# Block attention, experts and FFN on one core: host-made windows of keys and values, block means by VectorE and GpSimd

## What is computed

```python
B, H, S, D = q.shape
block, window = (32, 16)
nb = S // block                                   # 24
k_sum = k.reshape(B, H, nb, block, D).max(axis=3)
v_sum = v.reshape(B, H, nb, block, D).mean(axis=3)
scores_l = scale * np.matmul(q, k.transpose(0, 1, 3, 2))
mask_l = np.abs(pos[:, None] - pos[None, :]) < window
scores_s = scale * np.einsum('bhsd,bhnd->bhsn', q, k_sum) + np.log(block)
scores_all = np.concatenate([np.where(mask_l, scores_l, -1e9), scores_s], axis=-1)
a = softmax(scores_all)                           # denominator + 1e-9
out = np.matmul(a, np.concatenate([v, v_sum], axis=2))
```

## Time and profile before

| what | value |
|---|---|
| runs | 876.49, 880.53, 880.81 us (median 880.53) |
| profiled execution | span 878.4 us; its own time is not listed apart from the three runs |
| PE busy | 855.3 us, 97% of the span |
| DVE, ACT, POOL busy | 248.8, 222.3, 226.6 us |
| the chain that ended last | PE 94%, DMA 4%, ACT 1% |
| DMA | 47.34 MB, mean 54 GB/s, nearly all of the first 70 us at full load |

### The profile page before, as it was taken

One profiled execution on the slowest core, in us unless ns is written; L12 is line 12 of the kernel. 1 busy time (PEld: TensorE's weight loads), 2 busy tenths in 40 slices (PEclk: granted clock), 3 DMA queues, 4 the chain that ended last, 5 costly groups with the idle time before them and its releaser, 6 DMA issues.

```text
span 878.4 us, 11397 instructions
## 1 busy us (share of the span) xinstructions
PE 855.3 (97%) x4224; PEld 709.1 (81%) x4224; DVE 248.8 (28%) x582; ACT 222.3 (25%) x494; POOL 226.6 (26%) x155
## 2 busy tenths in 40 slices
PE   5779999999999999999999999999999999999998
PEld 4668888888888888888888888888888888888886
DVE  4875412121212121212121211112333333333333
ACT  3665611112201012201022202032512133312121
POOL 2345712034502034502034502227510023300000
PEclk9999999999999999999999999999999999999999
DMA  9996350002200002200002200003200002010101
GB/s 213 234 227 150 110 213 0 1 5 97 90 1 0 0 24 96 72 0 0 0 24 96 72 0 0 0 0 119 73 0 0 0 24 72 1 48 0 48 0 48
DMA packets 41400, 47.34 MB, mean 54 GB/s; under 512 B 14944, under 2 KB 32416, under 8 KB 41248
## 3 DMA queue, kind: packets, MB, share of 16 engines
q1 hardware_dynamic: 39168, 45.94, 18.4%
q10 hardware_dynamic: 2208, 1.08, 0.6%
HBM read 42.76 MB, written 3.17 MB: 52 GB/s over the span
## 4 chain that ended last, share of the span: by engine, by line
PE 94%; DMA 4%; ACT 1%; DVE 0%; SPq 0%; issue 0%; ACTq 0%; POOL 0%; DVEq 0%; POOLq 0%
PE bank L761 30%; PE bank L762 30%; PE bank L763 30%; DMA v_win<-v_win 3%; PE bank L738 2%; PE bank L753 1%; PE bank L719 1%; DMA v_raw<-v_rows 1%; PE bank L729 1%; ACT prob L442 1%; SPq L269 0%; ACTq L456 0%; POOL q_bd L344 0%; ACT v_win L452 0%; DVE k_max L563 0%
## 5 line engine op out<-in xcount | busy, mean ns | idle before, releaser
L761 PE MATMUL bank<-x_hi,w_hi 128*128 (+1 forms) x576 | 225.7, 392 | 0.0
L762 PE MATMUL bank<-x_hi,w_lo 128*128 (+1 forms) x576 | 224.4, 390 | 0.0
L763 PE MATMUL bank<-x_lo,w_hi 128*128 (+1 forms) x576 | 224.2, 389 | 0.0
L626 DVE SCALAR_TENSOR_TENSOR h_lo<-bank,h_hi 128x512 fp32r<-128x512 f32 x96 | 66.4, 691 | 356.4 <-ACT h_hi L489 356.4
L761 PE MATMUL bank<-h_hi,w_hi 128*128 128x512 f32 x384 | 149.4, 389 | 0.0
L763 PE MATMUL bank<-h_lo,w_hi 128*128 128x512 f32 x384 | 149.4, 389 | 0.0
L762 PE MATMUL bank<-h_hi,w_lo 128*128 128x512 f32 x384 | 149.4, 389 | 0.0
L365 POOL TENSOR_TENSOR w_lo<-stage,w_hi 128x1024 fp32r<-128x1024 f32 x40 | 96.8, 2437 | 162.2 <-ACT w_hi L473 162.2
L489 ACT ACTIVATE h_hi<-bank 128x512 fp32r<-128x512 f32 x96 | 56.9, 592 | 313.9 <-PE bank L763 313.9
L391 POOL TENSOR_TENSOR x_acc<-x_acc,y_tmp 128x512 f32 (+1 forms) x48 | 60.5, 1297 | 262.1 <-DVE y_tmp L646 262.1
L761 PEld LDWEIGHTS bank<-x_hi,w_hi 128*128 128x128 f32 x576 | 108.1, 188 | 23.5 <-issue 0.8
(11 more groups left out here) (48 smaller groups left out, 601.7 us busy)
## 6 DMA issues: line engine op xcount, KB each, us to landing
stage<-weights SPq DMA_DIRECT2D x48, 512.0 KB, 3.3
v_win<-v_rows SPq DMA_DIRECT2D x8, 480.0 KB, 4.8
k_raw<-k_t SPq DMA_DIRECT2D x8, 384.0 KB, 6.4
q_bd<-q_t SPq DMA_DIRECT2D x16, 192.0 KB, 6.0
v_raw<-v_rows SPq DMA_DIRECT2D x8, 384.0 KB, 7.9
p_bc<-p_rows SPq DMA_DIRECT2D x1, 3072.0 KB, 9.9
out<-p_bc SPq DMA_DIRECT2D x12, 256.0 KB, 2.0
v_win<-v_win ACTq DMA_DIRECT2D x8, 132.0 KB
```

What stands on the lines that cost most here:

```text
L626: nc.vector.scalar_tensor_tensor(h_lo[:, f % NH, :], h_bank(cc, f)[:], 0.0, h_hi[:, f % NH, :].bitcast(F32), ALU.max, ALU.subtract).then_i ...
L761: nc.tensor.matmul(dst, w_h, a_h, start=first, stop=False)
L762: nc.tensor.matmul(dst, w_l, a_h, start=False, stop=False)
L763: return nc.tensor.matmul(dst, w_h, a_l, start=False, stop=last)
```

## The change

The host lays out windows of keys (with 24 zero columns behind each) and of values, and values with features in partitions. Cut to its core:

```diff
 # host
-        "k_t": features_first(k),
-        "v_rows": v_rows,
+        "k_w": np.pad(windows(k_rows), ((0, 0), (0, 0), (0, 0), (0, NBLK))),
+        "v_t": v_rows,                      # now features_first(v)
+        "v_w": np.ascontiguousarray(windows(v_rows).transpose(0, 3, 2, 1)),
 # SBUF
-            k_win = sb(att, "k_win", [P, 2, TILES, KEYS])
-            k_raw = sb(att, "k_raw", [P, 2, SEQ])
-            v_raw = sb(att, "v_raw", [P, 2, SEQ // P, P])
+            k_win = sb(att, "k_win", [P, NK, TILES, KEYS])      # NK = 3
+            v_cols = sb(att, "v_cols", [P, 2, SEQ])
+            v_sum = sb(att, "v_sum", [P, 2, NBLK])
 # SP: load_keys, load_value_columns, load_value_windows
-                wait_count(sp, kcopy_done, len(RUNS) * (u - 1))
-                sp.dma_start(k_raw[:, u % 2, :], k_t[u, :, :]).then_inc(k_in[u % 2], 16)
+                wait_count(sp, scores_done, GROUPS * (u - NK + 1))
+                sp.dma_start(k_win[:, u % NK, :, :], k_w[u, :, :, :]).then_inc(k_in[u % NK], 16)
...
                 wait_count(sp, vsum_done, u - 1)
-                sp.dma_start(v_raw[:, u % 2, :, :], v[u, :, :].rearrange("(t p) n -> p t n", p=P)
-                             ).then_inc(vraw_in[u % 2], 16)
+                sp.dma_start(v_cols[:, u % 2, :], v_t[u, :, :]).then_inc(vcols_in[u % 2], 16)
...
                 wait_count(sp, pv_done, GROUPS * (u - 1))
-                for t0, nt in RUNS:
...
-                    sp.dma_start(v_win[u % 2][0:KW, t0:t0 + nt, :], src).then_inc(v_in[u % 2], 16)
+                sp.dma_start(v_win[u % 2][0:KW, :, :], v_w[u, :, :, :]).then_inc(v_in[u % 2], 16)
...
             load_keys(0)
             load_queries(0)
             sp.dma_start(cst[:], consts).then_inc(const_in, 16)
+            load_value_columns(0)
+            load_value_windows(0)
             load_keys(1)
             load_queries(1)
-            load_values(0)
-            load_value_windows(0)
+            load_value_columns(1)
+            load_value_windows(1)
+            load_keys(2)
             sp.dma_start(dp[:], probs.rearrange("(p t) e -> p t e", p=P)).then_inc(dp_in, 16)
-            load_keys(2)
-            load_values(1)
             for u in range(2, UNITS):
+                load_queries(u)
+                load_value_columns(u)
                 if u + 1 < UNITS:
                     load_keys(u + 1)
-                load_queries(u)
-                load_values(u)
-                load_value_windows(u - 1)
+                load_value_windows(u)
                 load_weights(0, u - 2)
-            load_value_windows(UNITS - 1)
 # POOL, slot 3u+2, behind normalize and spread_key_maxima
+            def spread_value_means(u, slot):
+                pool.wait_ge(vmean_done, u + 1)
...
+                nc.gpsimd.tensor_copy(means[:, 1:TILES, :], means[:, 0:1, :].broadcast_to([NBLK, TILES - 1, P])
+                                      ).then_inc(vrep_done, 1)
+                pool.wait_ge(vrep_done, u + 1)
 # ACT, slot 3u+2
                 nc.scalar.activation(v_win[u % 2][KW:KEYS, 0, :], ps_v[KW:KEYS, 0:P], ACT.Copy
                                      ).then_inc(vmean_done, 1)
-                act.wait_ge(vmean_done, u + 1)
-                act.dma_start(means[:, 1:TILES, :], means[:, 0:1, :].broadcast_to([NBLK, TILES - 1, P])
-                              ).then_inc(vrep_done, 16)
 # DVE: maxima now from k_win; key_windows (slot 3u-1) gone; value_sums new in slot 3u+1
-            def key_windows(u):
...
+            def value_sums(u):
+                dve.wait_ge(vcols_in[u % 2], 16 * (u // 2 + 1))
+                wait_count(dve, vturn_done, u - 1)
+                nc.vector.tensor_reduce(v_sum[:, u % 2, :], v_cols[:, u % 2, :].rearrange("p (n j) -> p n j", j=BLOCK),
+                                        AXIS.X, ALU.add).then_inc(vsum_done, 1)
 # PE, slot 3u+2 (C_MEAN: identity / 32)
-                for t in range(SEQ // P):
...
-                    last = nc.tensor.matmul(ps_v[KW:KEYS, 0:P], cst[:, at:at + NBLK], v_raw[:, u % 2, t, :],
-                                            start=(t == 0), stop=(t == SEQ // P - 1))
+                nc.tensor.matmul(ps_v[KW:KEYS, 0:P], v_sum[:, u % 2, :], cst[:, C_MEAN:C_MEAN + P],
+                                 start=True, stop=True).then_inc(vturn_done, 1)
```

More of the change, by code:

```diff
@@ L60 @@
 SLOTS = ALL_GROUPS + L_X
[L63 to L73, removed]
+NK = 3
+C_ID, C_MEAN, C_MASK = 0, P, 2 * P
+C_ALL = C_MASK + 3 * KEYS
 def constants():
@@ L83, in constants, with attention_moe_ffn @@
         at = C_MASK + kind * KEYS
-        key = np.arange(KW)[None, :] + window_start(t) - QT * t
-        c[:, at:at + KW] = np.where(np.abs(query - key) < WINDOW, 0.0, MASKED / SCALE)
+        key = np.arange(KW)[None, :] - WINDOW
+        seen = (np.abs(query - key) < WINDOW) & (key + QT * t >= 0) & (key + QT * t < SEQ)
+        c[:, at:at + KW] = np.where(seen, 0.0, MASKED / SCALE)
         c[:, at + KW:at + KEYS] = np.log(BLOCK) / SCALE
-    for blk in range(P // BLOCK):
-        c[BLOCK * blk:BLOCK * (blk + 1), C_AVG + NBLK - P // BLOCK + blk] = 1.0 / BLOCK
+    c[:, C_MEAN:C_MEAN + P] = np.eye(P, dtype=np.float32) / BLOCK
     return c
-def attention_moe_ffn(nc, consts, q_t, k_t, v, probs, weights, p_rows, out):
+def attention_moe_ffn(nc, consts, q_t, k_w, v_t, v_w, probs, weights, p_rows, out):
     ctx = ExitStack()
@@ L149, in attention_moe_ffn @@
         q_zeroed_low = sem("q_zeroed_low")
-        k_in = [sem(f"k_in{s}") for s in range(2)]
+        k_in = [sem(f"k_in{s}") for s in range(NK)]
         q_in = [sem(f"q_in{s}") for s in range(2)]
-        vraw_in = [sem(f"vraw_in{s}") for s in range(2)]
+        vcols_in = [sem(f"vcols_in{s}") for s in range(2)]
         v_in = [sem(f"v_in{s}") for s in range(2)]
         kmax_done = sem("kmax_done")
-        kcopy_done = sem("kcopy_done")
         kwin_done = sem("kwin_done")
@@ L348, in spread_key_maxima @@
                 pool.wait_ge(kmax_done, u + 1)
-                wait_count(pool, scores_done, GROUPS * (u - 1))
-                nc.gpsimd.tensor_copy(k_win[:, u % 2, :, KW:KEYS],
+                nc.gpsimd.tensor_copy(k_win[:, u % NK, :, KW:KEYS],
                                       k_max[:, u % 2, :].unsqueeze(1).broadcast_to([P, TILES, NBLK])
                                       ).then_inc(kwin_done, 1)
+            def spread_value_means(u, slot):
+                pool.wait_ge(vmean_done, u + 1)
+                pool.wait_ge(norm_done, slot - L_NORM + 1)
+                pool.wait_ge(kwin_done, min(u + 1, UNITS - 1) + 1)
+                for f, half in split_half(slot - 1, 1):
+                    pool.wait_ge(wlo_done if half else wlo_half, f + 1)
+                means = v_win[u % 2][KW:KEYS, :, :]
+                nc.gpsimd.tensor_copy(means[:, 1:TILES, :], means[:, 0:1, :].broadcast_to([NBLK, TILES - 1, P])
+                                      ).then_inc(vrep_done, 1)
+                pool.wait_ge(vrep_done, u + 1)
             def normalize(k):
@@ L373, in split_half_lo @@
                                                w_hi[:, f, cols].bitcast(F32), ALU.subtract)
-                if half == 1:
-                    last.then_inc(wlo_done, 1)
+                last.then_inc(wlo_done if half else wlo_half, 1)
             for slot in range(SLOTS + 1):
@@ L383, in _ @@
                     spread_key_maxima(u)
+                for u in unit_starting(slot, L_MEAN):
+                    spread_value_means(u, slot)
                 for f, half in split_half(slot, 1):
@@ L672, in _ @@
                     key_maxima(u)
-                for u in unit_starting(slot, -1):
-                    key_windows(u)
+                for u in unit_starting(slot, 1):
+                    value_sums(u)
                 if slot == L_TRANS:
@@ L845, in features_first, with windows @@
                                     ).reshape(UNITS, P, SEQ)
-    v_rows = np.ascontiguousarray(v.reshape(BATCH, KT, 2, SEQ, DH).transpose(0, 1, 3, 2, 4)
-                                  ).reshape(UNITS, SEQ, P)
+    def windows(a):
+        padded = np.pad(a, ((0, 0), (0, 0), (WINDOW, WINDOW)))
+        return np.stack([padded[:, :, QT * t:QT * t + KW] for t in range(TILES)], axis=2)
+    k_rows, v_rows = features_first(k), features_first(v)
     halves = F2 // FE
@@ L868 @@
     out = nc.dram_tensor("out", (TOK, DM), F32, kind="ExternalOutput").ap()
-    attention_moe_ffn(nc, ap["consts"], ap["q_t"], ap["k_t"], ap["v_rows"], ap["probs"], ap["weights"],
+    attention_moe_ffn(nc, ap["consts"], ap["q_t"], ap["k_w"], ap["v_t"], ap["v_w"], ap["probs"], ap["weights"],
                       p_rows, out)
```

41 lines of the change are left out of this document (17 added, 24 removed).

## The result

| | runs, us | median | ratio to the kernel before, 95% interval |
|---|---|---|---|
| before | 876.49, 878.12, 880.53, 880.81 | 879.33 | |
| changed | 883.80, 884.33, 884.84, 885.33 | 884.59 | 1.0058 (1.0034 to 1.0081) |

The changed kernel is slower by 5.3 us. Its profiled execution has a span of 882.0 us and took 883.80, so 1.8 us lie outside the span; the spans differ by 3.6 us.

What follows compares the result with a forecast made beforehand. PE was taken as the bound, so only the first 105 us could move: -7.2 us by slot 19, -2.4 from units 6 and 7, +0.5 for half clock, rounded to -9: 880.5 - 9.0 = 871.5 us; range 866.5 to 880.

Steps and rivals of the forecast that it cites:

- the steps of the start: Start, unit 0: second keys' maxima at 14.3 instead of 9.57 us, ACT's copy done at 22.7 instead of 20.1, +2.6 us.
- the end of the wait for the spread: Values' wait for the DMA spreading means over v_win, 7.57 to 9.05 us of transfer, goes altogether.
- PE's means: Two matmul records replace twelve, 0.24 us instead of 1.42 a unit; sure for units 6 and 7, -2.4 us.
- the first landmark: End of unit 0's last values group: 30.8 us, against 28.2 before; 29.7 with a quicker spread and faster rows.
- GpSimd's copy: POOL's spread of means, 24 partitions by 1408 columns: 2.05 us, between 1.3 and 4.4.
- SP now blocks on values: SP's wait in load_value_windows(u) makes a loop through units 1 to 3: period 9.5 us, bounds 9.0 to 10.4.
- The queries' landing: In SP's loop, issue, windows, weights and queries: landed 6.8 us after values end, 8.2 if all at 230 GB/s.
- PE's three steps: Scores, transposing and values after the queries land, ending the unit: 2.2 us at full clock.
- The engines' own period: Time of a unit without a DMA wait, 9.0 us from the old kernel's last; lower bound of the loop.
- Queries come late: Rival, chance 0.07: landing takes 9.3 us, PE's next steps run at half clock, period 14.9; 890.6 us, slower.
- Only bytes count: Rival, chance 0.13: all DMA rows move at 233 GB/s, a unit takes 11.3 us; 879.6 us, no change.
- The spread is the wait: Rival, chance 0.10: POOL's copy needs 4.4 us, disturbed by DVE's reductions, period 10.5; 876.3 us.

Runs made afterwards that it cites:

- the fastest version: Changed kernel, second keys loaded ahead of first value columns and windows; SP's loop asks for windows(u-1) right after queries(u), ahead of keys: 866.79 us, ratio 0.9864.

## Why the prediction was wrong

**Right:** where the time is decided (before slot 19; PE without a gap from there but for 0.97 us), the steps of the start (maxima of unit 1 at 14.31 against 14.3, sums, first mask, spread, and ACT's copy done at 22.7 as added up), VectorE's prices, and the end of the wait for the spread. PE's means take 0.33 us a unit on the chain, not 0.24, so they save 1.1 and not 1.2.

That the first landmark came out at 30.77 against 30.8 is luck in part. Three experiments leave the loads of the start as they are, and in their profiled executions unit 0 ends at 29.9, 31.9 and 34.0 us. The second keys' maxima scatter with it. The changed kernel, the earliest and the latest of them:

```profile
14.31 0.95 DVE L559 TENSOR_REDUCE k_max<-k_win 128x24 f32<-128x768 f32 x1 [7.52 <-DMA k_win<-k_w]
...
13.50 0.95 DVE L561 TENSOR_REDUCE k_max<-k_win 128x24 f32<-128x768 f32 x1 [6.71 <-DMA k_win<-k_w]
...
16.56 0.95 DVE L559 TENSOR_REDUCE k_max<-k_win 128x24 f32<-128x768 f32 x1 [9.75 <-DMA k_win<-k_w]
```

Inside the start, the exponents came 0.5 us later than added up, and the shorter spread made up for it.

GpSimd's copy was nearer the lower bound, 1.36 instead of 2.05 us: I had drawn a line from one short copy through zero, while 0.42 at 288 and 1.36 at 1408 columns leave 0.84 ns a column and 0.2 us fixed. (The lower bound of 1.3 doesn't follow from half of 2.05 ns, which gives 1.45 for 1408 columns.) GPSIMD Engine Reference in the Trainium skill (Performance versus the Vector engine) puts a loop bound by its ports at 1.03 cycles an element and counts with 1.2 GHz; that gives 0.86 ns, an estimate, and the trace agrees with 0.84.

The forecast was 871.5 us, 9 less than before; measured were 884.59, 5.3 more. **The step that failed** is "SP now blocks on values", a period of 9.5 from bounds of 9.0 and 10.4. The loop was the right one, wait by wait; it took 12.1, 13.2 and 13.6 us. Two of its terms were too small.

- *The queries' landing*, put at 6.8 us after the wait, 8.2 at most; measured 8.0, 9.1 and 9.6. The DMA view of the second turn, 42.8 to 44.5 and 44.5 to 52 us:

```profile
DMA packets 17, 0.10 MB, mean 61 GB/s; under 512 B 0, under 2 KB 0, under 8 KB 17
...
DMA packets 1991, 2.03 MB, mean 271 GB/s; under 512 B 1615, under 2 KB 1615, under 8 KB 1991
```

From the wait's end to the landing at 52 us the queues moved 2.13 MB; windows, weights and queries are 1.51. The other 0.6 MB can only be value columns and first keys, issued behind the queries but moved beside them. I had counted only what stands ahead. 0.62 MB at this rate is 2.3 us, and 271 instead of the 302 GB/s that my terms imply is 0.6 more; 0.10 MB moved before 44.5 takes back 0.4. That is 2.5 us, and the measured excess is 2.3.

DMA: Bandwidth & Descriptors in the Trainium skill (Queues, rings and completion order) says that completion isn't first in, first out for an issuing engine. The trace agrees in two of four turns. In the third the weights, issued at 56.39 us, and the first half of the queries, issued behind them at 56.86, landed this much later, at 63.7 and 63.2:

```profile
stage<-weights SPq DMA_DIRECT2D x1, 512.0 KB, 7.3
q_bd<-q_t SPq DMA_DIRECT2D x1, 192.0 KB, 6.3
```

- *PE's three steps*, put at 2.2 us, took 4.0 at the half clock (1.2 GHz) behind waits of 3.5 to 4.1 us. I had given the clock 0.5 us in all, outside the loop. Inside it, it is paid in every turn: 5.6 us by the experiment that kept PE busy.

Together 1.2 to 2.8 and 1.8 us a turn on top of the lower bound of 9.0: 12.9 in the mean instead of 9.5, 10.2 us at unit 3. Slots 17 and 18 took 8.9 instead of 7.3, the first at the half clock. Slot 19 began at 78.38, not 66.6. From there the means gave 2.2 of the 2.4, and 0.97 was lost where PE waited for x_lo, whose VectorE stood behind maxima waiting for keys: 4.6 - 2.2 + 1.0 = 3.4 of the spans' 3.6 us.

The engines' own period, taken as 9.0 from the old kernel, was too long besides: the fastest version has 7.5, 8.6 and 9.0 us. So the loop cost the changed kernel about 4.5 us a turn.

**The rivals.** "Queries come late" was the case, given 0.07; the period of 12.9 us lies past its threshold of 11.9, and its 890.6 had the landing too late. (Its own terms, with 10.8 us from unit 3 to slot 19, give no change at 11.5 and the 4.4 us at 13.0; the 11.9 doesn't follow from them.) I had argued against it from the longest landing seen and from how many packets stood ahead. That was the wrong reading: the loop needs no long landing, since every microsecond of it is paid three times with PE's clock on top. "Only bytes count" wasn't the cause, since bytes were the same in all loop orders, and the fastest version moves 285 to 295 GB/s, not 233. "The spread is the wait" was wrong: the spread took 1.36 us, not 4.4.

## What to carry to other kernels

Asking sooner can be later. Before an order of loads is judged by its bytes, follow the queue that issues them: a wait for a late stage ahead of loads that an early stage needs ties both into a loop, and each of its terms is paid every turn. Price such a loop with everything issued behind the wait up to the landing, also what stands behind the load in question, and with PE's steps at the clock that its idle time leaves. A part's worth depends on the bound: the same padded keys cost 4 us where DMA was full and gave 5 where VectorE was.

## Not expected of the hardware

- 16 needless fp32 matmuls three times made the kernel 5.6 us faster, because the clock stayed at 1.00.
- After a wait of 3.52 us, 8 records of scores took 2.06 us at half clock, against 1.15 at full clock. In another run a wait of 2.14 us cost no clock, and one of 2.09 did (2.03).
- The same loads in the same order at the start: the second keys' maxima began at 13.50, 14.31, 14.74 and 16.56 us in four executions of four versions.
- The old kernel with its value windows asked for one step of SP's loop sooner, and nothing else, went from 879.88 to 898.25 us.
